# Two of seven taps on GpSimd in the convolutions of the second, third and fourth piece

## The reference, cut to what matters

```python
# x (4, 4096, 192), weight_gen (4, 4096, 8 heads, 7 taps), all float32
w = softmax(weight_gen, axis=-1)                  # over the 7 taps, sum + 1e-9
x_pad = concatenate([zeros of 6 positions, x])    # along the sequence
out[b,s,h,g] = sum over k of w[b,s,h,k] * x_pad[b, s+k, h, g]    # h: 8 heads of 24 channels
h = out.reshape(16384, 192) @ w_in                # 192 x 2048
g = h * (1 / (1 + exp(-1.702 * h)))
result = g @ w_out                                # 2048 x 192, float32
```

## Time and profile before

| | kernel before |
|---|---|
| time, median of 3 runs (lowest to highest) | 1124.35 us (1123.55 to 1124.76) |
| the profiled execution: its time | 1123.73 us |
| its span in the trace | 1122.0 us |
| TensorE busy / VectorE / ScalarE / GpSimd | 1115.6 / 801.1 / 620.9 / 11.7 us |
| mean granted TensorE clock | 1.00 (2.4 GHz) |
| one unit of TensorE | 4.31 us |

### The profile page before, as it was taken

One profiled execution on the slowest core, in us unless ns is written; L12 is line 12 of the kernel. 1 busy time (PEld: TensorE's weight loads), 2 busy tenths in 40 slices (PEclk: granted clock), 3 DMA queues, 4 the chain that ended last, 5 costly groups with the idle time before them and its releaser, 6 DMA issues.

```text
span 1122.0 us, 21780 instructions
## 1 busy us (share of the span) xinstructions
PE 1115.6 (99%) x9788; PEld 922.4 (82%) x9788; DVE 801.1 (71%) x710; ACT 620.9 (55%) x662; POOL 11.7 (1%) x16
## 2 busy tenths in 40 slices
PE   9999999999999999999999999999999999999998
PEld 7888888888888888888888888888888888888886
DVE  8899988586685966859668596785858768587322
ACT  7768664464645546455564554645555555454543
POOL 2100000000000000000000000000000000000000
PEclk9999999999999999999999999999999999999999
DMA  8801010101001010010100101010010100100000
GB/s 259 245 8 54 15 54 1 40 29 40 29 1 40 29 40 29 3 58 9 40 29 32 38 1 40 30 40 30 1 40 29 40 30 1 40 29 1 30 1 29
DMA packets 9836, 43.00 MB, mean 38 GB/s; under 512 B 1104, under 2 KB 2640, under 8 KB 7440
## 3 DMA queue, kind: packets, MB, share of 16 engines
q1 hardware_dynamic: 8256, 40.44, 10.8%
q0 software_dynamic: 1488, 1.18, 0.8%
HBM read 24.71 MB, written 12.58 MB: 33 GB/s over the span
## 4 chain that ended last, share of the span: by engine, by line
PE 99%; DVE 0%; issue 0%; ACTq 0%; DVEq 0%; POOL 0%; ACT 0%; POOLq 0%
PE hid L691 47%; PE acc_main L707 31%; PE acc_rest L707 21%; PE acc_main L628 1%; PE hid L632 0%; PE acc_main L747 0%; PE acc_main L653 0%; DVE outs_rest L594 0%; PE acc_rest L747 0%; DVE outs_main L525 0%; ACTq L74 0%; PE acc_rest L653 0%; DVEq L74 0%; POOL gate_lo L599 0%; ACT outs_main L366 0%
## 5 line engine op out<-in xcount | busy, mean ns | idle before, releaser
L323 ACT ACTIVATE gate<-hid 128x1024 f32<-128x1024 f32 x256 | 263.3, 1028 | 479.7 <-PE hid L691 479.1
L577 DVE TENSOR_TENSOR gate_lo<-gate,gate_hi 128x1024 fp32r<-128x1024 f32 x256 | 313.0, 1223 | 260.4 <-ACT gate_hi L331 258.4
L691 PE MATMUL hid<-xt,w_hi 64*128 64x512 f32 x3072 | 430.9, 386 | 0.0
L691 PEld LDWEIGHTS hid<-xt,w_hi 64*128 64x128 f32 x3072 | 288.1, 184 | 60.4 <-ACT xt L303 0.2
L707 PE MATMUL acc_main<-gate_hi,w 64*128 64x512 f32 x2032 | 313.2, 386 | 0.0
L331 ACT ACTIVATE gate_hi<-hid 128x1024 fp32r<-128x1024 f32 x254 | 258.6, 1018 | 0.0
L707 PEld LDWEIGHTS acc_main<-gate_hi,w 64*128 64x128 f32 x2032 | 190.5, 184 | 39.8
L691 PE MATMUL hid<-xt,w_lo 64*128 64x512 f32 x1536 | 216.1, 386 | 0.0
L707 PE MATMUL acc_rest<-gate_lo,w 64*128 64x512 f32 x1016 | 198.0, 386 | 0.0
L707 PE MATMUL acc_rest<-gate_hi,w 64*128 64x512 f32 x1016 | 198.0, 386 | 0.0
L707 PE MATMUL acc_main<-gate_lo,w 64*128 64x512 f32 x1016 | 198.0, 386 | 0.0
(11 more groups left out here) (76 smaller groups left out, 253.0 us busy)
## 6 DMA issues: line engine op xcount, KB each, us to landing
xwin<-in_x_runs SPq DMA_DIRECT2D x15, 1056.0 KB, 4.8
out<-outs_main SPq DMA_DIRECT2D x13, 512.0 KB, 2.6
out<-outs_rest SPq DMA_DIRECT2D x13, 256.0 KB, 2.9
taps<-in_tap_runs SPq DMA_DIRECT2D x1, 3136.0 KB, 12.7
taps<-in_w_rows SPq DMA_DIRECT2D x2, 1536.0 KB, 9.7
w_hi<-w_hi SPq DMA_DIRECT2D x2, 768.0 KB, 9.8
w_lo<-w_lo SPq DMA_DIRECT2D x2, 768.0 KB, 8.0
out<-outs_main SPq DMA_DIRECT2D x6, 256.0 KB, 2.2
```

Of the source, the lines that this page charges most:

```text
L323: nc.scalar.activation(gate[:, v % 2, :, :], hid[:, v % 2, :, :], ACT.Gelu_apprx_sigmoid).then_inc(gate_ready, 1)
L577: nc.vector.tensor_tensor(gate_lo[:, v % SLOTS, :, :], gate[:, v % 2, :, :], gate_hi[:, v % SLOTS, :, :], ALU.subtract).then_inc(gate_lo_r ...
L691: last = nc.tensor.matmul(hid[:, v % 2, h, :], w[rows, k if j else slice_of(h, k), q, f], xt[rows, j % 2, part, k, :], start=(i == 0), sto ...
```

## The change

GpSimd gets new work for the narrow pieces 1, 2 and 3: the products of taps 5 and 6 and their sum. They are put into the upper halves of the two prod buffers (help_prod), which narrow pieces leave free after the head. VectorE keeps taps 0 to 4 and their four sums, and adds GpSimd's sum as the last step ("join", L435 of the changed kernel), which waits for the semaphore help_summed. Its list for a narrow piece has 10 steps in place of 13; the rows of STEPS_AT for pieces 0, 1 and 2 are shorter by 3, 4 and 2 steps, and the list stands at the same step again when the wide pieces begin.

```diff
--- before.py
+++ after.py
@@ -23,9 +23,9 @@
 W1_ADDED_AT = 4
 MAX_AT, EXP_AT = 2, 3
 
-STEPS_AT = ((0, 5, 3, 2, 2, 2, 4, 2),
-            (3, 4, 4, 2, 4, 6, 0, 5),
-            (1, 2, 0, 6, 3, 4, 1, 2),
+STEPS_AT = ((0, 5, 3, 2, 2, 2, 1, 2),
+            (3, 4, 3, 2, 3, 5, 0, 4),
+            (1, 2, 0, 5, 2, 4, 1, 2),
             (0, 2, 1, 2, 2, 1, 4, 1),
             (0, 0, 1, 2, 3, 0, 2, 2, 1, 0, 2, 1, 2, 1, 2, 0))
 ROUND_AT = (7, 5, 5, 7, 12)
@@ -34,6 +34,7 @@
 CROSS_HI_AT, CROSS_LO_AT = (7, 7, 5), (7, 7, 5)
 WARM_UP = 16
 SHARED = 3
+HELPED = 2
 
 
 def ffn_of_dynamic_conv(nc: bass.Bass, x_runs: bass.AP, tap_runs: bass.AP, x_first: bass.AP, tap_first: bass.AP,
@@ -112,6 +113,7 @@
         head_sum = prod[:, 1, N_FIRST:N_CONV]
         shared_prod = [conv[:, 0:N_FIRST], conv[:, N_FIRST:N_CONV], head_more[:]]
         zeros = gate_lo[:, 0, 0, 0:P].bitcast(F32)
+        help_prod = [prod[:, i, NARROW * CB:N_CONV] for i in range(HELPED)]
         head_flat = outs_main[:].rearrange("p h n -> p (h n)")
 
         head_conv = head_flat.rearrange("p (u k c) -> p u k c", k=SLICES + 1, c=HALF)
@@ -140,6 +142,7 @@
         w2_negated, w2_added, w2_late_ready = sem("w2_negated"), [sem("w2_added_soon"), sem("w2_added_late")], sem("w2_late_ready")
         taps_maxed, taps_shifted, taps_exped = sem("taps_maxed"), sem("taps_shifted"), sem("taps_exped")
         conv_op, conv_ready = sem("conv_op"), sem("conv_ready")
+        help_op, help_summed = sem("help_op"), sem("help_summed")
         turned_ready = sem("turned_ready")
         xt_hi_ready, xt_lo_ready = sem("xt_hi_ready"), sem("xt_lo_ready")
         hid_ready = sem("hid_ready")
@@ -371,21 +374,24 @@
                     nc.scalar.activation(outs_rest[:, h, cols], acc_rest[HALF:P, h, cols], ACT.Copy).then_inc(rest_crossed, 1)
 
         SOFTMAX_STEPS = 4
-        ORDER = [("mul", 0), ("mul", 1)]
-        for k in range(2, K):
-            ORDER += [("mul", k), ("add", k - 1)]
-        ORDER += [("add", K - 1)]
-        CONV_STEPS = SOFTMAX_STEPS + len(ORDER)
-        STEPS = CONV_STEPS + 2
-
-        STREAM = [(1, q) for q in range(STEPS)] + [(2, q) for q in range(STEPS - 1)]
+        def order(own_taps):
+            steps = [("mul", 0), ("mul", 1)]
+            for k in range(2, own_taps):
+                steps += [("mul", k), ("add", k - 1)]
+            return steps + [("add", own_taps - 1)]
+
+        ORDER = [order(K - HELPED) + [("join", K - 1)] if is_narrow(j) else order(K) for j in range(LAST + 1)]
+        CONV_STEPS = [SOFTMAX_STEPS + len(steps) for steps in ORDER]
+        OP0 = [sum(CONV_STEPS[1:j]) - (j - 1) for j in range(LAST + 1)]
+
+        STREAM = [(1, q) for q in range(CONV_STEPS[1] + 2)] + [(2, q) for q in range(CONV_STEPS[2] + 1)]
         for j in range(3, LAST + 1):
-            STREAM += [(j, q) for q in range(SOFTMAX_STEPS)] + [(j - 1, STEPS - 1)]
-            STREAM += [(j, q) for q in range(SOFTMAX_STEPS, STEPS - 1)]
-        STREAM += [(LAST, STEPS - 1)]
+            STREAM += [(j, q) for q in range(SOFTMAX_STEPS)] + [(j - 1, CONV_STEPS[j - 1] + 1)]
+            STREAM += [(j, q) for q in range(SOFTMAX_STEPS, CONV_STEPS[j] + 1)]
+        STREAM += [(LAST, CONV_STEPS[LAST] + 1)]
 
         def conv_step(dve, j, q):
-            base = (j - 1) * (CONV_STEPS - 1)
+            base = OP0[j]
             u = PIECES[j]
             g = u * HB
             t = taps[:, tap_span(j, j)].rearrange("p (g k) -> p g k", k=K)
@@ -405,7 +411,7 @@
                 nc.vector.tensor_tensor(norm, t, tap_inv[:, 0:g].unsqueeze(2).broadcast_to([P, g, K]), ALU.mult
                                         ).then_inc(conv_op, 1)
             else:
-                what, k = ORDER[q - SOFTMAX_STEPS]
+                what, k = ORDER[j][q - SOFTMAX_STEPS]
                 if what == "mul":
                     if k == 0:
                         if j == 1:
@@ -423,9 +429,14 @@
                                             xwin[:, at:at + u, :].rearrange("p t (h c) -> p (t h) c", c=GRP),
                                             norm[:, :, k:k + 1].broadcast_to([P, g, GRP]), ALU.mult
                                             ).then_inc(conv_op, 1)
+                elif what == "join":
+                    dve.wait_ge(conv_op, base + q)
+                    dve.wait_ge(help_summed, j)
+                    nc.vector.tensor_tensor(acc, acc, help_prod[0], ALU.add).then_inc(conv_ready, 1)
                 else:
                     last = k == K - 1
-                    dve.wait_ge(conv_op, base + q - (not last))
+                    closing = k == K - 1 - (HELPED if is_narrow(j) else 0)
+                    dve.wait_ge(conv_op, base + q - (not closing))
                     nc.vector.tensor_tensor(acc, acc, prod[:, k % 2, 0:u * CB], ALU.add
                                             ).then_inc(conv_ready if last else conv_op, 1)
 
@@ -465,9 +476,9 @@
             def prepare(first, last):
 
                 for j, q in STREAM[first:last]:
-                    if q < CONV_STEPS:
+                    if q < CONV_STEPS[j]:
                         conv_step(dve, j, q)
-                    elif q == CONV_STEPS:
+                    elif q == CONV_STEPS[j]:
                         turn_piece(j)
                     else:
                         split_piece(j)
@@ -612,12 +623,40 @@
                                         ).then_inc(shared_op, 1)
             pool.wait_ge(w1_negated, 1)
             pool.dma_start(w1_raw[:, :, LATE], w1_lo[:, :, 0, LATE].bitcast(F32), accum_op=ALU.add).then_inc(w1_added, 16)
+
+            def help_multiply(j):
+                pool.wait_ge(conv_op, OP0[j] + SOFTMAX_STEPS)
+                if j == 1:
+                    pool.wait_ge(head_summed, SLICES + 1)
+                    pool.wait_ge(x_added, 16)
+                else:
+                    pool.wait_ge(x_reloaded, 16)
+                    pool.wait_ge(conv_ready, j - 1)
+                u = PIECES[j]
+                g = u * HB
+                norm = tap_norm[:, 0:g * K].rearrange("p (g k) -> p g k", k=K)
+                for i in range(HELPED):
+                    k = K - HELPED + i
+                    at = k + (NARROW if j == 3 else 0)
+                    nc.gpsimd.tensor_tensor(help_prod[i].rearrange("p (g c) -> p g c", c=GRP),
+                                            xwin[:, at:at + u, :].rearrange("p t (h c) -> p (t h) c", c=GRP),
+                                            norm[:, :, k:k + 1].broadcast_to([P, g, GRP]), ALU.mult).then_inc(help_op, 1)
+
+            def help_add(j):
+                pool.wait_ge(help_op, HELPED * j)
+                nc.gpsimd.tensor_tensor(help_prod[0], help_prod[0], help_prod[1], ALU.add).then_inc(help_summed, 1)
+
+            help_multiply(1)
             for i, (at, to) in enumerate(LATE_CHUNKS):
                 pool.wait_ge(w2_negated, i + 1)
                 for q in range(2):
                     pool.dma_start(w2_of(at, to, slice(0, D), w2_raw)[:, q],
                                    w2_of(at, to, slice(D, 2 * D)).bitcast(F32)[:, q], accum_op=ALU.add
                                    ).then_inc(w2_added[i], 16)
+            help_add(1)
+            for j in (2, 3):
+                help_multiply(j)
+                help_add(j)
 
         @block.tensor
         def _(pe):
```

## The result

The changed kernel takes 1132.24 us (median of 6 runs, 1131.92 to 1133.66) against 1124.38 us (6 runs, 1123.55 to 1124.76): 7.9 us slower, ratio 1.0073 (95% interval 1.0063 to 1.0083). The profiled execution took 1132.77 us, its span is 1131.0 us, 9.0 more than before.

The account below looks back on a forecast made before the run. The prediction took TensorE alone to bound the kernel. Stalls of 1.4, 2.3 and 0.8 us in pieces 1, 2 and 3, together 4.5, on the profiled 1123.73 gave 1128.2 us; range 1123.5 to 1131.0.

Parts of the forecast that it names:

- The bound, and what goes: TensorE alone bounds the kernel; VectorE losing three instructions net per piece, 7.8 us in all, is worth nothing.
- (a): VectorE's join waiting for GpSimd's sum: in piece 1 the sum ends 2.5 us before the join, so no wait.
- (b): DMAs for w2 behind GpSimd's products start at 29.3 instead of 28.66 us and land 4.3 us after issue: hidden.
- The disputed cost: GpSimd beside VectorE instructions with two SBUF operands: from no loss to VectorE standing still 4.5 us a piece.
- the far end: The two engines take turns: VectorE stands still for each GpSimd instruction, 4.5 us a piece, less what slack hides.
- the nearest row: GpSimd's products in the head beside VectorE's with one SBUF operand, 0.95 us against 0.96 elsewhere: VectorE loses nothing.
- The sum, piece 1: Stall in piece 1: one, two, three GpSimd instructions ahead of gate_lo of units 2, 3, 4; largest counts, 1.4 us.
- Pieces 2 and 3: Stalls of 2.3 us in piece 2 and, with one GpSimd product ahead of unit 6's gate_lo, 0.8 in piece 3.
- The range: The measured time would lie from 1123.5 to 1131.0 us, taking in no contention, contention within the slack and the forecast.
- my upper case: A second GpSimd product also ahead of the gate_lo of unit 6 in piece 3: 1.5 us more, up to 1131.

Follow-up runs that it names:

- run 1: The changed kernel without GpSimd's products and sum and without the join's wait, taps 5 and 6 left out of pieces 1 to 3: 1123.94 us.
- run 4: The changed kernel with GpSimd's sum for piece 1 ahead of the four DMAs for w2 instead of behind them: 1134.74 us.
- run 2: The kernel before plus nine GpSimd products on an SBUF scratch tile at the change's places, nobody waiting for them: 1135.74 us.
- run 3: The kernel before plus two GpSimd memsets, which only write SBUF, at each place of the change's GpSimd instructions: 1124.39 us.
- run 8: The changed kernel, but GpSimd's sum for piece 1 starts only when the first pair of DMAs for w2 has landed: 1130.00 us.
- run 7: The changed kernel cut down so that GpSimd helps piece 3 alone, pieces 1 and 2 as before: 1128.19 us.
- run 5: The changed kernel cut down so that GpSimd helps piece 1 alone, pieces 2 and 3 as before: 1129.81 us.
- run 6: The changed kernel cut down so that GpSimd helps piece 2 alone, pieces 1 and 3 as before: 1128.02 us.
- run 9: The changed kernel helping piece 1 alone, GpSimd's work started after the first w2 DMA pair landed, the join one unit later: 1124.33 us.
- run 12: The kernel before plus nine GpSimd tensor_scalar instructions, each reading one operand from an SBUF scratch tile, nobody waiting for them: 1130.60 us.
- run 10: The changed kernel with each GpSimd product and sum cut into two of 128x384: 1132.67 us.

## Why the prediction was wrong

- **The bound, and what goes**: right. TensorE had nothing to gain; run 1 shows it (1123.94 us).
- **New waits (a), (b)**: the join never waited in the changed kernel, and the DMAs stayed hidden, as forecast. The margin of (b) was too wide: it used 4.3 us from issue to landing, and run 4, in which the DMAs start 2.1 us later than in the changed kernel, shows 10.1.
- **The disputed cost**: the mechanism was right, and the choice of the far end against the nearest row with it. Runs 2 and 3 show that it is the reads. The 1.5 us for each product were 1.35.
- **The sum, piece 1**: this step failed. It gave 1.4 us, and 4.0 were measured. I had put one GpSimd instruction ahead of the gate_lo of unit 2; both products came (2.7 - 1.20 = 1.5, measured 1.6). I had put two ahead of unit 3's; the sum came beside it as the third. And I had priced that sum at 1.5 us; behind the four DMA issues it held VectorE off for 2.96 (2.7 + 3.0 - 1.78 = 3.9, measured 4.0). Runs 8 and 2 show that this is its place and not its kind: started later it holds 1.65, and in run 2 a product at that place holds 2.61.
- **Pieces 2 and 3**: 2.3 and 0.8 forecast, 3.1 us together; from unit 1 to unit 6, 4.15 were lost (23.65 - 19.50). For piece 2 the price was right: with the clock at full it is 2.0 before unit 2 and 0.3 before unit 3 (run 4). For piece 3 a step failed: "One GpSimd product fits in front", it says of the gate_lo of unit 6. Both did, and the forecast's own price for two is 2.3; run 4 has 1.7. The 0.4 of the changed kernel looks like a hit of the 0.8 only because TensorE came there late by the clock; that is luck. The relief of VectorE did count: without it, piece 3 costs 2.4 us or more (run 7). The slacks here were also read 0.16 us too large, since the chain of the earlier trace rows puts a call's start where the matmul before it ends; the timeline has 63.95, 68.26 and 79.14 us.
- **The clock**: no term had it, and in the profiled execution TensorE lost 1.7 us while it was down. The total did not need the term, as unit 6 waits for VectorE with it or without it. The rows of before, with the clock at 1.00 in each stretch, did not show that a stall can lower it; runs 5 to 7 do, and there it costs 1.4 to 1.9 us.
- **The range**: it ended at 1131.0 us; my upper case added only a second product in piece 3. 2.6 us in piece 1 and 1.0 in pieces 2 and 3 were missing: 1128.2 + 3.6 = 1131.8, with the 0.6 us between the profiled execution and the median 1132.4, where 1132.24 was measured.

## What to carry to other kernels

Before work goes to GpSimd, list what VectorE runs beside it: an instruction with two operands in SBUF and a GpSimd instruction that reads SBUF take turns, so the offload does not add an engine there, and what VectorE is held off costs what exceeds the slack at the next hand-over, to be summed over all that comes before it. Where the bounding engine never waits, relieving another one is worth nothing, and each new stall is paid in full. Where TensorE stands still for 2 us, a loss of clock can follow (1.4 to 1.9 us here); it adds to the time only if TensorE does not wait for VectorE again further on.

## What the runs showed of the hardware that was not expected

- A GpSimd instruction that started while DMAs of its queue were still being issued held VectorE off for once, about twice or three times its usual time, in the order in which it started before their end. Started 0.4 us before it, a product held its usual 1.35 us (run 9); 0.9 before, a product held 2.61 for 1.27 (run 2); 1.1 before, the sum held 2.96 for 1.65 (changed kernel; 1.65 in runs 8 and 9); 1.9 before, a one-operand instruction held 1.9 us in three shares, for 0.64 (run 12). Why is open.
- TensorE's clock fell to half for 3.4 us behind stalls of 1.8 to 2.5 us (changed kernel, runs 4, 7, 8, 10) and for 6.8 us behind one of 3.3 (run 2); it did not fall behind others of 1.8 to 2.1 us (changed kernel, runs 4, 5, 6, 12). By the mean clock it fell in 3 of 4, 6 of 10 and 5 of 9 runs of kernels 5 to 7. What decides whether it falls was not found.
- GpSimd's tensor_scalar on 128x768 took 2.4 us beside VectorE, longer than its product of two tensors of that size at the same place (1.8 us).
